# Sink probabilities transposed once per head pair, against three variants of the sink values

## The reference

```python
# q, k, v: 4 batches, 8 heads, 768 positions, 64 columns
scores = scale * np.matmul(q, k.transpose(0, 1, 3, 2))
pos = np.arange(S)
is_sink = pos[None, :] < int(n_sink)                     # the first 4 positions
rel = pos[:, None] - pos[None, :]
in_window = (rel >= 0) & (rel < int(window))             # the last 128
scores = np.where(is_sink | in_window, scores, -1000000000.0)
scores = scores - np.max(scores, axis=-1, keepdims=True)
a = np.exp(scores)
a = a / (np.sum(a, axis=-1, keepdims=True) + 1e-09)
attn_out = np.matmul(a, v)
# then h = x @ w_in; x = (h - np.tanh(h)) @ w_out; then the experts
```

## Time and profile before

| | |
|---|---|
| time, median of 3 runs | 1068.89 us (1068.62 to 1070.78) |
| span of the profiled execution | 1067.3 us |
| busy in it | PE 986.2 us (92%), DVE 699.5 (66%), ACT 612.0 (57%), POOL 400.9 (38%) |
| the chain that ended last | PE 64%, DVE 19%, issue 5%, ACT 5%, DMA 3%, POOL 2% |
| the sinks' transposes on PE (L662) | 96 of 128x128 in f32 |
| the sinks' product on PE (L709) | 32 of 128x384 in f16 |

### The profile page before, as it was taken

The page is one execution under the profiler, slowest core; times in us unless marked ns, Lnnn a source line. Parts: engine busy times, 40 slices in busy tenths (PEclk is TensorE's granted clock), DMA queues, the critical chain, the costliest instruction groups (busy, mean ns, idle before and its releaser), DMA issues.

```text
span 1067.3 us, 24226 instructions
## 1 busy us (share of the span) xinstructions
PE 986.2 (92%) x7776; PEld 624.8 (59%) x7776; DVE 699.5 (66%) x2464; ACT 612.0 (57%) x1425; POOL 400.9 (38%) x462
## 2 busy tenths in 40 slices
PE   1668999999999999999899999999899999899996
PEld 0534555655565565556466556555487777677773
DVE  6677977668978867877876885637665334733331
ACT  2677887757766866767676776536412224522221
POOL 4788898213344412325522341011122322232322
PEclk9767999999999999999999999999999999999998
DMA  8943113311411333211231130051025111111111
GB/s 237 328 130 71 36 36 77 120 36 37 100 36 36 65 97 71 66 36 36 40 97 36 36 65 2 1 188 31 9 43 207 53 49 44 39 41 49 49 49 38
DMA packets 25165, 75.22 MB, mean 70 GB/s; under 512 B 10032, under 2 KB 10416, under 8 KB 23536
## 3 DMA queue, kind: packets, MB, share of 16 engines
q1 hardware_dynamic: 16176, 60.65, 21.1%
q0 software_dynamic: 5728, 13.43, 3.9%
q10 hardware_dynamic: 3168, 0.02, 0.2%
HBM read 60.23 MB, written 14.12 MB: 70 GB/s over the span
## 4 chain that ended last, share of the span: by engine, by line
PE 64%; DVE 19%; issue 5%; ACT 5%; DMA 3%; POOL 2%; DVEq 1%; SPq 1%; ACTq 0%; POOLq 0%
PE h_ps L750 16%; PE acc L806 15%; PE pt_ps L1846 10%; PE h_ps L1897 5%; PE acc L1897 5%; DVE qk_top L400 3%; DVE g_raw L771 2%; PE x_out L707 2%; PE pt_ps L645 2%; PE s_ps L575 2%; PE s_ps L857 2%; DVE pt_lo L632 1%; DVE g_lo L791 1%; DMA qk_raw<-in_qk 1%; DVE ew_lo L1542 1%
## 5 line engine op out<-in xcount | busy, mean ns | idle before, releaser
L806 PE MATMUL acc<-w_out_all,g_hi 128*128 128x512 f16 x768 | 228.4, 379 | 0.0
L750 PE MATMUL h_ps<-xt_hi,w_in_all 128*128 128x384 f16 x960 | 196.7, 328 | 14.7 <-DVE g_raw L771 14.6
L806 PE MATMUL acc<-w_out_all,g_lo 128*128 128x512 f16 x384 | 145.8, 380 | 4.6 <-DVE g_lo L791 2.8
L750 PEld LDWEIGHTS h_ps<-xt_hi,w_in_all 128*128 128x128 f16 x960 | 91.7, 98 | 84.2 <-DVE g_raw L771 18.9
L628 ACT ACTIVATE pt_hi<-pt_ps 128x256 f16<-128x256 f32 (+1 forms) x192 | 69.1, 360 | 114.3 <-PE pt_ps L645 113.6
L100 POOL TENSOR_TENSOR tick<-tick 1x1 f32<-1x1 f32 x83 | 16.0, 193 | 276.2 <-ACT y L1913 118.3
L806 PEld LDWEIGHTS acc<-w_out_all,g_hi 128*128 128x128 f16 x768 | 75.0, 98 | 70.2
L791 DVE SCALAR_TENSOR_TENSOR g_lo<-g_raw,batch_scale,g_hi 128x384 f16<-128x384 f32 x128 | 90.0, 703 | 34.9 <-ACT g_hi L781 33.5
L451 POOL TENSOR_TENSOR q_stack<-qk_raw,q_stack 64x768 f16<-64x768 f32 x31 | 51.1, 1650 | 164.3 <-ACT q_stack L447 164.3
L781 ACT ACTIVATE g_hi<-g_raw,batch_scale 128x384 f16<-128x384 f32 x128 | 78.1, 610 | 39.4 <-DVE g_raw L771 39.3
L608 ACT ACTIVATE normed<-probs,row_sum 128x260 f32<-128x260 f32 (+1 forms) x192 | 92.8, 484 | 12.0 <-DVE row_sum L603 11.6
(11 more groups left out here) (310 smaller groups left out, 2109.0 us busy)
## 6 DMA issues: line engine op xcount, KB each, us to landing
qk_raw<-in_qk SPq DMA_DIRECT2D x62, 454.0 KB, 6.0
raw<-in_w SPq DMA_DIRECT2D x16, 512.0 KB, 7.9
v_raw<-in_v SPq DMA_DIRECT2D x4, 1536.0 KB, 9.2
x_tokens<-x SPq DMA_DIRECT2D x24, 256.0 KB, 5.7
w_in_all<-in_w_in SPq DMA_DIRECT2D x4, 1024.0 KB, 13.0
w_out_all<-in_w_out SPq DMA_DIRECT2D x4, 1024.0 KB, 12.0
x_tokens<-g_raw SPq DMA_DIRECT2D x1, 1024.0 KB, 13.7
qk_raw<-in_qk SPq DMA_DIRECT2D x2, 262.0 KB, 4.4
```

What stands on the lines that cost most here:

```text
L750: mm = eng.matmul(h_of(m, f), w16[0][:, f, x * DM + k * P:x * DM + (k + 1) * P], r[:, par, k, :], start=(i == 0), stop=(i == 3 * KD - 1))
L806: mm = eng.matmul(acc[t][:, :], l[f % 2][:, t * P:(t + 1) * P], w16[1][:, f, x * DM:(x + 1) * DM], start=(f == 0 and i == 0), stop=(f == N ...
```

## The change

The sinks' probabilities are transposed once, with all 24 rows of a strip in use, so that they take one block of `pt_hi` and not three. The values take three variants, one for each query tile, with their 8 rows at 0, 8 or 16 of each strip and zero elsewhere. Each tile's columns of `x_out` get a product of their own.

```diff
-    vs_raw = sb("vs_raw", [P, DM], F32)
-    vs_all = [sb(f"vs_all{s}", [P, DM], F16) for s in range(2)]
+    vs_raw = sb("vs_raw", [P, TPC, DM], F32)
+    vs_all = [sb(f"vs_all{s}", [P, TPC, DM], F16) for s in range(2)]
...
-    sinks = sb("sinks", [P, 4 * SINK + P], F32)
-    pt_hi, pt_lo = (sb(n, [P, 12 + TPC, P], F16) for n in ("pt_hi", "pt_lo"))
+    sinks = sb("sinks", [P, P], F32)
+    pt_hi, pt_lo = (sb(n, [P, 12 + 1, P], F16) for n in ("pt_hi", "pt_lo"))
...
-                for strip in range(3):
-                    for hh in range(2):
-                        src = dram["v"][b, 0:SINK, 0:DM].rearrange("s (g c) -> s g c", c=P)[:, :, D * hh:D * hh + D]
-                        row = STRIP * strip + SINK * (1 - hh)
-                        dst = vs_raw[row:row + SINK, :].rearrange("s (g c) -> s g c", c=P)[:, :, D * hh:D * hh + D]
-                        eng.dma_start(dst, src).then_inc(q["vs_in"], 16)
+                for t in range(TPC):
+                    for strip in range(3):
+                        for hh in range(2):
+                            src = dram["v"][b, 0:SINK, 0:DM].rearrange("s (g c) -> s g c", c=P)[:, :, D * hh:D * hh + D]
+                            row = STRIP * strip + SINK * (2 * t + 1 - hh)
+                            dst = vs_raw[row:row + SINK, t, :].rearrange("s (g c) -> s g c", c=P)[:, :, D * hh:D * hh + D]
+                            eng.dma_start(dst, src).then_inc(q["vs_in"], 16)
...
-                eng.wait_ge(q["vs_in"], 96 * (b + 1))
+                eng.wait_ge(q["vs_in"], 16 * 6 * TPC * (b + 1))
                 eng.tensor_scalar(vs_raw[:], vs_raw[:], v_scale[:, b, 0:1], 1.0, ALU.mult, ALU.mult).then_inc(q["vs_mult"], 1)
...
-                low = vs_all[s][STRIP:2 * STRIP, :]
-                eng.tensor_tensor(low, vs_raw[STRIP:2 * STRIP, :], low, ALU.subtract).then_inc(q["vs_lo_done"], 1)
+                low = vs_all[s][STRIP:2 * STRIP]
+                eng.tensor_tensor(low, vs_raw[STRIP:2 * STRIP], low, ALU.subtract).then_inc(q["vs_lo_done"], 1)
...
-                for t in range(TPC):
-                    first = 2 * SINK * t
-                    mm = eng.transpose(out[:, t, :], sinks[:, first:first + P], ident[:])
-                mm.then_inc(q["transposed"], 1)
+                eng.transpose(out, sinks[:], ident[:]).then_inc(q["transposed"], 1)
...
-                eng.activation(pt_hi[:, 12:12 + TPC, :], out, ACT.Copy).then_inc(q["pt_hi_done"], 1)
+                eng.activation(pt_hi[:, 12, :], out, ACT.Copy).then_inc(q["pt_hi_done"], 1)
...
-                low = pt_hi[0:STRIP, 12:12 + TPC, :]
+                low = pt_hi[0:STRIP, 12, :]
...
-                    mm = eng.matmul(x_out.rearrange("p (t c) -> p t c", t=TPC), vs_all[par][:, hp * P:(hp + 1) * P],
-                                    pt_hi[:, 12:12 + TPC, :], start=False, stop=True, skip_group_check=True)
+                    for of_t in range(TPC):
+                        mm = eng.matmul(x_out[:, of_t * P:(of_t + 1) * P], vs_all[par][:, of_t, hp * P:(hp + 1) * P],
+                                        pt_hi[:, 12, :], start=False, stop=True, skip_group_check=True)
```

More of the change, by code:

```diff
@@ L109, in attention_buffers @@
     v_hi, v_lo = ([sb(f"v_{x}{s}", [P, NB2 * HP, VW], F16) for s in range(2)] for x in ("hi", "lo"))
-    vs_raw = sb("vs_raw", [P, DM], F32)
-    vs_all = [sb(f"vs_all{s}", [P, DM], F16) for s in range(2)]
+    vs_raw = sb("vs_raw", [P, TPC, DM], F32)
+    vs_all = [sb(f"vs_all{s}", [P, TPC, DM], F16) for s in range(2)]
     probs = sb("probs", [P, RING, KW], F32)
     normed = sb("normed", [P, 6, KW], F32)
-    sinks = sb("sinks", [P, 4 * SINK + P], F32)
-    pt_hi, pt_lo = (sb(n, [P, 12 + TPC, P], F16) for n in ("pt_hi", "pt_lo"))
-    words = 4 * QK + 2 * CT + 4 * KR + NB2 * DM + 2 * NB2 * HP * VW + 2 * DM + RING * KW + 6 * KW + 4 * SINK + P + 15 * P
+    sinks = sb("sinks", [P, P], F32)
+    pt_hi, pt_lo = (sb(n, [P, 12 + 1, P], F16) for n in ("pt_hi", "pt_lo"))
+    words = 4 * QK + 2 * CT + 4 * KR + NB2 * DM + 2 * NB2 * HP * VW + 2 * TPC * DM + RING * KW + 6 * KW + P + 13 * P
     return (qk_raw, q_stack, kh_stack, kl_stack, v_raw, v_hi, v_lo, vs_raw, vs_all, probs, normed, sinks, pt_hi, pt_lo), words
@@ L655, in transpose_sinks @@
             m = 7 * g + 6
-            out = pt_bank[m % 2][:, 0:CT].rearrange("p (t c) -> p t c", t=TPC)
+            out = pt_bank[m % 2][:, 0:P]
             if E == "pe":
```

## The result

The changed kernel takes 1077.62 us (median of 4 runs, 1075.98 to 1080.85), the kernel before 1069.40 beside it (4 runs, 1068.62 to 1070.78): a ratio of 1.0081, 95% interval 1.0065 to 1.0097. The change costs about 0.8%, where 1067.5 was forecast. The profiled execution spans 1075.4 us, 8.1 more than before.

The account below looks back on a forecast made before the run. Other engines set the pace at the start, then PE bounds a long stretch. Start +5.1, alone stage -1.3, window 0 +0.9, windows 2 and 4 +0.2, pairs -6.25 gave about -1.4 us: 1067.5 us, range 1064.2 to 1071.8.

Parts of the forecast that it names:

- the pairs: Windows' head pairs: two transposes fewer, products unchanged, -0.22 us PE each over 25 pairs; with DVE's L671, -6.25 us.
- dearer-products rival: Sink products in each pair: 0.083 us a step if weight loads aren't hidden; +0.65 us, 1069.6; chance 0.10.
- the start: Before pair two's scores: wider multiply +0.86, wider low half +1.94, twelve more loads +2.3; +5.1 us (bounds 3.9 and 6.8).
- the alone stage: Attention alone, before the windows: pairs three and four give back 1.3 us, so the windows start 3.8 us late.
- wide bounds: Landing of the twelve extra loads at the start: between 1.1 and 4.0 us, 2.3 taken.
- windows 2 and 4: Sink values of later batches made there: no weight splits behind ACT's copy, so +0.1 us each.
- POOL's own 1.94 us lies behind the multiply: Window 0: POOL's longer low half stands ahead of the same wait for ACT; nothing added for it.
- window 0: ACT late by wider multiply and copy, delaying PE's wait on L361: +0.9 us (bounds 0 and 1.5).
- slower rival: Loads hold POOL: start 6.8 us, no give-back from pairs three and four, window 0 1.5; +2.2 us, 1071.1; chance 0.14.
- PE time turns into waiting: Windows: half of the pairs' 5.5 us PE gain returns as waits on g_raw; +1.4 us, 1070.3; chance 0.12.

Follow-up runs that it names:

- e5: Changed kernel with the low half of the sink values (32x1536) on DVE instead of POOL; 1083.45 us, ratio 1.0135 to the kernel before.
- s2: Changed kernel with one strip per query tile, one load a batch, low half in three DVE operations; 1078.73 us, ratio 1.0100 to the kernel before.
- s6_variants_by_act: Changed kernel with one strip per tile, one load, one 512-column POOL subtraction, variants filled by three ACT copies; 1065.01 us, ratio 0.9968 to the kernel before.
- s3_variants_spread: Changed kernel with one strip per tile, one load, variants filled by three POOL subtractions at separate slots; 1067.12 us, ratio 0.9995 to the kernel before.

## Why the prediction was wrong

**The parts add up.** Pairs -0.58%, loads +0.25%, low half +0.50%, multiply and copy +0.54%: +0.71% for the sum of the four ratios, and +0.81% measured for the whole. The intervals of the parts, 0.15 to 0.20% to either side each, rule out only a large interaction, and there is one in the small: the hold in window 2 costs 1.4 us with the low half alone and 2.6 with the wide copy beside it.

**Right: the pairs.** Forecast -0.22 us on PE each; measured -0.21, with three products at 0.18 us together. L293's 0.057 us a product holds (0.18 / 3 is 0.06) and the dearer-products rival falls. The Trainium skill's figure of about 81 ns ("TensorE: Matmul & The Clock Gate", "Back-to-back issue gap") is for a sustained stream; three in a row, the case here, would take 0.24 us by it, an estimate, and the trace doesn't agree. ACT's copy takes 272 ns, DVE's low part 269. The windows were to shrink by 6.25; with the pairs' part alone the way from the first MLP matmul to the last pair's product is 5.8 us shorter (604.12 to 598.29), and 1061.9 us is the price of the change without its values.

**Right: the start.** +5.3 us at pair two for 5.1, and 1.7 given back by the alone stage for 1.3: first MLP matmul at 94.02 for 94.2. The loads' 2.5 us hit the middle of wide bounds (2.3), but by luck and not by my reasoning. I let SP issue the twelve more in 4.1 us, all before the queue reaches them. In fact four of the issues take 0.56 to 1.95 us, and the weight group behind them is issued at 25.98, where 22.3 was forecast. How much of a landing is the receipt no run shows.

**Wrong: windows 2 and 4.** The step that failed is "Windows 2 and 4 have no weight splits, so nothing of that kind stands behind the copy: +0.1 each". It looked for what is queued behind the longer operations, and found nothing; the cost comes from another engine's operation that runs beside them. In window 2 the hold of g_lo costs 2.6 us, in window 4 2.1 and the lower clock 1.5 more, in place of 0.1 each. The same blind spot is in the term "POOL's own 1.94 us lies behind the multiply": it was weighed as POOL's time alone, which ends in a wait of POOL for ACT, and POOL was busy only 44% of windows 2 and 4 before. So the part with the largest rise in duration was costed at nothing in all three windows.

**Wrong: window 0**, +0.9 (bounds 0 and 1.5). The mechanism named is there: ACT waits 1.82 us for the multiply, PE waits 1.53 for ACT's normalisation and 1.95 for L361 (forecast 2.3 on L361 alone). The term was mis-sized: by the matched matmuls PE loses 3.4 us from 173 to 186, 0.9 of it a wait on a held g_lo of 3.00 us (timeline of PE):

```profile
178.23 0.39 PE L805 MATMUL acc<-w_out_all,g_lo 128*128 128x512 f16 x1 [0.88 <-DVE g_lo L790]
```

Another 1.7 us are the lower clock at 123.7, which no term covered.

**The clock.** Both places lie at a wait of PE on g_raw (1.19 and 1.82 us). The kernel before has such waits too, two of 1.82 us, which end at 338.48 and 512.72, and keeps the higher level there. In the profiled executions of the thirteen kernels this wait of 1.82 us stands 26 times between 100 and 700 us, and the lower level begins at 5 of them; it begins at all six of the longer waits on g_raw in e5 and s2 (2.48 to 4.56 us). What decides at 1.82 us I can't say. That the changed kernel meets two such places in its profiled execution and the pairs' part alone none is measured, that its moved waits cause them isn't shown. The clock may have a share in the median too: the mean granted clock is 0.968 to 0.979 in the four executions of the kernel after, 0.974 to 0.985 in seventeen of the kernel before. How much of the 0.8% that is the runs don't show.

**The rivals.** None of mine was the right one. The slower rival had its place at the start, and its price, +2.2, was a quarter of the real loss. "PE time turns into waiting" had the right form, but named g_raw, whose waits stay (12.5 us for 13.0), and not g_lo.

**What it sums to.** Against the forecast's -1.4 us: start and alone stage -0.2, pairs +0.4, window 0 +2.5 at the sink values, +1.7 by the clock and -0.3 ahead of both, window 2 +2.5, window 4 +2.0 and the clock +1.5, window 3 +0.5 (DVE waits 1.86 us for a load of keys, 0.82 before, and PE for DVE), and -1.1 behind the beginning of window 7: +9.5, the measured difference (8.1 + 1.4).

## What to carry to other kernels

An operation that gets longer on an engine with room isn't free by that alone: look on the other engines for operations that lie under it, and compare their longest execution with their median. Here one row of the kernel before, 1.11 us for an operation with a median of 0.62, told the price of making POOL's operation three times as long. Where a long GpSimd operation can't be avoided, cut it into pieces or give the work to ScalarE, under whose operations alone no g_lo lasted over 0.64 us. Pieces help only as far as their new places meet nothing: with all steps in pieces, holds of 2.76 us came up elsewhere. Don't move the operation to the engine that PE waits for: behind the new wait stands all that is queued there.

## What the runs showed of the hardware that I had not expected

- A DVE operation with two SBUF operands doesn't get through until the computing operation of POOL that was running when it began has ended: g_lo, 0.62 us alone, lasts 3.11 and ends 0.42 us behind it, and an operation on 24 columns, 0.18 alone, lasts 2.16 and ends 0.04 behind it. Between two operations of POOL it may get its turn (1.17 us, low half in three pieces) or be held over three of them (2.76 us, steps spread); what decides that I can't say. If DVE is first by as little as 0.07 us, it isn't held, and POOL's operation can last longer instead (3.44 for 3.09). POOL's tensor_scalar operations hold too (1.53 us at most beside L428); its indirect DMAs don't (seven executions of g_lo beside them in the kernel after, all 0.61 or 0.62). A copy with one SBUF operand, 0.21 us alone, was held for up to 1.17.
- SP's issue of a small load takes about 0.30 us for the first eleven of the eighteen, then 0.56, 1.20, 1.95 and 0.93, then 0.30 again: 9.77 us in all, where six took 2.06. What holds those four the trace doesn't say.
- The twelve runs of s6_variants_by_act and of s3_variants_spread spread over 7 us each, as much as the effects in question, so one profiled execution alone places a kernel badly. The mean granted clock goes with it loosely: the two fastest of s6_variants_by_act show 0.983, the slowest 0.975.
